# The last low part of the next expert's second weight moves behind the low parts of its rows on VectorE

## The reference

```
for e in range(E):                      # E = 8
    mask = e_idx == e                   # each active token has one expert
    if not mask.any():
        continue
    h = np.maximum(xc[mask] @ w1[e], 0.0)
    y[mask] = gate_w[mask, None] * (h @ w2[e])
out[do_compute] = xc + y
```

## Time and profile before

| | us |
|---|---|
| timed runs, median of 3 | 1353.08 |
| timed runs, lowest and highest | 1351.26, 1353.22 |
| the profiled execution | 1349.94 |
| its span | 1348.1 |
| PE busy in the span | 1313.8 (97%) |
| DVE busy in the span | 844.6 (63%) |
| ACT busy in the span | 566.4 (42%) |

### The profile page before, as it was taken

One profiled execution on the slowest core, in us unless ns is written; L12 is line 12 of the kernel. 1 busy time (PEld: TensorE's weight loads), 2 busy tenths in 40 slices (PEclk: granted clock), 3 DMA queues, 4 the chain that ended last, 5 costly groups with the idle time before them and its releaser, 6 DMA issues.

```text
span 1348.1 us, 24739 instructions
## 1 busy us (share of the span) xinstructions
PE 1313.8 (97%) x9435; PEld 760.2 (56%) x9435; DVE 844.6 (63%) x1487; ACT 566.4 (42%) x868; POOL 291.4 (22%) x251
## 2 busy tenths in 40 slices
PE   6999999999999999999999999999999999999987
PEld 3776667655455456445545644654564465556665
DVE  5999999686576247436634742762464375568983
ACT  5999999642134114304312420440242043226662
POOL 3667666623002000300300030030003000121211
PEclk9999999999999999999999999999999999999999
DMA  9344441051011011001101100100110122468940
GB/s 239 94 115 110 107 114 52 20 205 63 1 63 63 1 63 62 0 0 65 59 0 62 62 0 17 72 36 0 62 62 0 43 79 82 155 216 296 343 154 21
DMA packets 51632, 109.84 MB, mean 81 GB/s; under 512 B 5216, under 2 KB 8840, under 8 KB 51568
## 3 DMA queue, kind: packets, MB, share of 16 engines
q1 hardware_dynamic: 48880, 105.40, 24.8%
q0 software_dynamic: 2240, 3.35, 0.7%
q10 hardware_dynamic: 448, 0.19, 0.1%
HBM read 93.57 MB, written 17.34 MB: 82 GB/s over the span
## 4 chain that ended last, share of the span: by engine, by line
PE 92%; DVE 3%; ACT 2%; issue 1%; DMA 1%; SPq 1%; POOL 0%; ACTq 0%; POOLq 0%; DVEq 0%
PE ps L1673 14%; PE ps L1676 14%; PE ps L1677 14%; PE ps L1699 11%; PE ps L1702 11%; PE ps L1701 11%; PE ps L1596 5%; PE ps L1584 2%; PE ps L1586 2%; PE ps L1568 2%; PE ps L1606 1%; PE ps L1608 1%; PE ps L1610 1%; ACT probsT_hi L811 1%; DMA qk_in<-kT 1%
## 5 line engine op out<-in xcount | busy, mean ns | idle before, releaser
L1699 PE MATMUL ps<-x_hi,w_hi 128*128 128x384 f16 x896 | 292.1, 326 | 1.9 <-DVE parts L1254 1.1
L1702 PE MATMUL ps<-x_hi,w_lo 128*128 128x384 f16 x896 | 292.1, 326 | 0.0
L1701 PE MATMUL ps<-x_lo,w_hi 128*128 128x384 f16 x896 | 292.1, 326 | 0.0
L1677 PE MATMUL ps<-w_hi,h 128*128 128x512 f16 x768 | 291.0, 379 | 0.0
L1676 PE MATMUL ps<-w_lo,h 128*128 128x512 f16 x768 | 291.0, 379 | 0.0
L1673 PE MATMUL ps<-w_hi,h 128*128 128x512 f16 x768 | 291.0, 379 | 0.0
L1311 DVE SCALAR_TENSOR_TENSOR x<-ps,gate_now,x 128x512 f32<-128x512 f32 x84 | 63.1, 751 | 251.7 <-PE ps L1677 250.8
L927 ACT ACTIVATE x1s<-ps 128x384 f32<-128x384 f32 x64 | 30.4, 475 | 327.3 <-PE ps L1702 327.3
L625 POOL TENSOR_TENSOR wf<-wf 128x1024 f32<-128x1024 f32 x8 | 18.8, 2354 | 633.4 <-PE ps L1702 622.5
L944 ACT ACTIVATE h<-parts 128x1152 f16<-128x1152 f32 x64 | 74.4, 1163 | 141.4 <-DVE parts L1269 141.4
L1677 PEld LDWEIGHTS ps<-w_hi,h 128*128 128x128 f16 x768 | 75.1, 98 | 90.6
(11 more groups left out here) (228 smaller groups left out, 2235.7 us busy)
## 6 DMA issues: line engine op xcount, KB each, us to landing
wf<-w1a SPq DMA_DIRECT2D x32, 512.0 KB, 6.0
w_stage_in<-w2a SPq DMA_DIRECT2D x8, 2048.0 KB, 8.9
w_in<-w1b SPq DMA_DIRECT2D x4, 2048.0 KB, 9.6
w_in<-w2b SPq DMA_DIRECT2D x4, 2048.0 KB, 9.6
w_in_b<-w1b SPq DMA_DIRECT2D x4, 2048.0 KB, 10.2
w_in_b<-w2b SPq DMA_DIRECT2D x4, 2048.0 KB, 10.0
rows<-blank SPq DMA_DIRECT2D x1, 6682.0 KB, 21.5
qk_in<-kT SPq DMA_DIRECT2D x32, 192.0 KB, 4.5
```

The source lines that it names most:

```text
L1677: last = pe.matmul(acc, a_lo, b_hi, start=False, stop=(m == n - 1))
L1699: pe.matmul(group_bank(g, role), w_hi, x_hi, start=(opens and kt == 0), stop=False, skip_group_check=not opens)
L1701: pe.matmul(group_bank(g, role), w_hi, x_lo, start=False, stop=False, skip_group_check=not opens)
L1702: last = pe.matmul(group_bank(g, role), w_lo, x_hi, start=False, stop=(kt == 1), skip_group_check=not opens)
```

## The change

In `own_expert` of DVE the fourth quarter of `w2`'s low part is taken out of the loop and placed behind the two row tiles of the next expert. It holds for experts 1 to 6; expert 7 has no next one. No other engine's program is changed.

```diff
             def own_expert(e):
                 for n in range(PARTS):
                     hidden_pair(CAP, 4 * e, n)
-                    if e + 1 < E:
+                    if e + 1 < E and n < PARTS - 1:
                         own_w2_part(e + 1, n)
                 if e + 1 < E:
                     for k in range(CS):
                         turn_row_tile(k, CS * (e + 1) + k + 1)
+                    own_w2_part(e + 1, PARTS - 1)
                 if e + 2 < E:
                     for n in range(PARTS):
                         own_w1_part(e + 2, n)
```

## The result

The changed kernel takes 1345.09 us (median of 6; 1343.41 to 1345.89) against 1352.4 us before (median of 6; 1349.28 to 1353.5). The ratio is 0.9952, 95% interval 0.9939 to 0.9965: 4.7 to 8.2 us faster, where the forecast was 1.1. Measured again on another occasion, the ratio was 0.9951 (0.9937 to 0.9965). The profiled execution took 1345.64 us.

What follows compares the result with a forecast made beforehand. DVE was taken to set the pace up to expert 3's hidden layer, PE from there. Terms: -1.13 us in expert 2, 0 elsewhere, so 1353.08 - 1.13 = 1351.95 us; range 1348.5 to 1354.5.

Steps and rivals of the forecast that it cites:

- Expert 2: Hand-over from expert 2 to 3: PE's first hidden-layer matmul waits less for `xgT_lo`, so it comes 1.13 us sooner.
- The high part's cover: ACT's `xgT_hi` is ready before DVE needs it: by 0.5 us in expert 1, 2.5 us in expert 2; later idle costs nothing.
- The moved `w_lo`: It ends 1.20 us later, delaying SP's next `w2` load into that buffer; 8 us of cover before ACT reads it.
- 0 elsewhere: Hand-overs other than expert 2's: PE wasn't waiting for `xgT_lo`, so nothing to win; smallest cover 0.8 us, in expert 4.
- the mechanism as a rival: Expert 5's hidden layer: PE's code arrives sooner against expert 7's `w2` load, hole closes, up to 5.7 us, 1346.3; chance 0.15.
- the likeliest case: Whole kernel: forecast as worked out, 1.13 us won in expert 2 and 0 elsewhere, 1351.95 us; chance 0.67.
- The wait that isn't there in timed runs: Expert 3's start: in timed runs PE comes 1.1 us later, `xgT_lo` is hidden anyway, no change, 1353.1; chance 0.10.
- A new hole: PE from expert 3 on: another code page comes late against shifted `w2` loads, up to 5.7 us, 1357.6; chance 0.08.

## Why the prediction was wrong

**Expert 2** was right to the digit: 1.13 us in the changed kernel's profile, and the gap of 0.33 us that is left is the 0.21 and 0.12 worked out. **The high part's cover** held: in expert 1 no idle appeared on DVE ahead of `xgT_lo`, and in expert 3 there was 0.23 us of it, at no cost to PE:

```profile
1271.49 1.29 DVE L1382 SCALAR_TENSOR_TENSOR xgT_lo<-ps,xgT_hi 128x512 f16<-128x512 f32 x2 [0.23 <-ACT xgT_hi L993]
```

**The moved `w_lo`** is the step that failed, and with it the term "0 elsewhere" of the sum: the hole of 5.81 us in expert 5 closed. I followed the later load only to its reader, ACT, found 8 us of cover and put the effect at nothing. The load's readers never mattered. What mattered is what else is fetched by the same DMA engines while it runs: a block of PE's own code. I had the mechanism as a rival, at its price of 5.7 us (measured: 5.81), and gave it 0.15. So the step's result was wrong, and the chance with it. The size of the shift between load and PE was about right (1.2 us worked out, 1.3 measured, 1.96 to 0.66), but my words tied it to PE's gain in expert 2, though in the bracket that gain falls out on both sides. The trace with the swap in expert 2 alone shows that load and PE move together with that gain; the shift comes from the swap in expert 4 itself, where 1.20 us of `xgT_lo` stand ahead of the low part that releases the load, and it comes in every run with that swap. I also missed that the tiles, moved forward, bring the code request 1.03 us sooner against PE, which adds to it. That a shift of this size is enough couldn't be read off the trace of before; how long the packet takes when nothing is ahead of it, about 1 us, could.

The rule of the Trainium skill that I set against this rival ("DMA: Bandwidth & Descriptors", section "Queues, rings and completion order") says that a DMA engine takes its queues in turn, packet by packet. My reading of it, that the load would hardly hold up a fetch, is refuted: the hole grows with the load, 1.28, 2.89 and 4.03 us, so the measurement decides. The rule itself may stand: it allows packets of up to 64 descriptors, and this load's 1024 pieces of 2 KB are 64 for each of the 16 engines, if they are spread evenly. How many make a packet here, no run shows. The other ("Runtime: NRT & Kernel Launch", section "Instruction fetch mechanics": code in blocks, a taken branch breaks the prefetch) agrees with the packet's 16 KB and with the hole that moves by as many matmuls as were put ahead. That a branch starts it wasn't tried; the packet's fixed distance from the wait just ahead of one fits it.

**"0 elsewhere"** had a second gap: the covers in the other hand-overs were measured behind a hole of 5.8 us. With the hole closed PE comes sooner, the cover of expert 5 to 6 is gone, and the swap there, which I had costed at nothing, is worth the 1.08 us that the swap in expert 4 alone shows. So the change is three terms: 1.1 us in expert 2; 5.8 us of hole and low clock in expert 5, of which 1.0 comes back in waits for `rh_lo` and the step behind them; and 1.1 us not lost from 5 to 6. The third is a loss avoided, which the kernel before hadn't either, so it isn't in the sum: 1.13 + 0.11 + 5.81 - 1.03 = 6.0 us between the profiles, inside the 4.7 to 8.2 measured. My rival's own time, 1346.3, stood close to the median of 1345.09, in part by luck, since it left the 1.03 out and the median before had been 0.7 us lower by then (1352.4); the likeliest case and the range were off.

**The wait that isn't there in timed runs** isn't settled by the swap in expert 2 alone (ratio 0.9996, so 0.8 us slower to 1.9 faster). The changed kernel and the one with experts 4 and 5 differ by some 2 us in the direction of a wait that is there, with intervals that overlap. **A new hole** on top of the old didn't come in the changed kernel.

## What to carry to other kernels

When a step is moved that releases a DMA, look at everything that shares the DMA engines in the new and the old window, code fetches above all, and not only at who reads the loaded data. Look too at what the steps that come sooner release: here the same swap brought the code request forward. A stop of PE named "issue" between two matmuls of one loop, with an instruction packet landing just ahead of the restart, costs what it lasts plus the low clock after it, and a later issue of one large load can remove it. And read the covers of the other hand-overs again with the hole taken out, since the engine that comes sooner uses them up.

## What the hardware showed beyond that

A code packet, once begun, is over in about 1 us, alone (0.96 in the changed kernel) or in the midst of the load (1.04 in the kernel before). What the load takes from it is the time until it begins: 5.95 us after the load's issue in the kernel before (1295.27), and PE went on 1.4 us after its end (1296.32). After the hole PE ran at half pace: the second part of that hidden layer had its matmuls 0.11 us apart for a while the earlier trace rows. The same low clock shows up elsewhere without any change of code: the hidden layer that begins near 1222, ahead of all swaps and behind a wait for rows, takes 5.31 us in the profile of the kernel before, 6.71 in the changed kernel's, and 8.1 in that with the swap in expert 2 alone. The changed kernel's row for it:

```profile
1222.00:1229.50 7.50, 7.45 (x103) 7.46 (x104) 4.74 (x5) 2.23 (x4) 1.67 (x2) 0.80 0.98 347
```

One to three such microseconds are of the size of the spread among runs of one kernel, so that single profiles were compared here only from expert 1's results on.
